# Two half-height products for the remainder rows of the last layer's first two matrices, on one Trainium2 core

## What is computed

```python
def _moe2_ref(x, w_a, w_b, w_out):        # x 3072 x 320, w_a and w_b 320 x 1536, w_out 1536 x 320
    a = x @ w_a
    b = x @ w_b
    return (a * b @ w_out).astype(np.float32)
```

## Time and profile before

| what | value |
| --- | --- |
| median of 3 runs | 934.4 us (932.12 to 934.41) |
| the profiled execution's own time | 929.12 us |
| its span, first to last instruction | 927.4 us |
| granted TensorE clock, mean of the span | 0.948 of full speed |
| TensorE busy | 811.5 us, 88% of the span |
| DVE busy | 612.4 us, 66% |
| ACT busy / POOL busy | 287.4 us / 168.8 us |
| matmuls of `wide` on wa and wb | 480 + 288 for each of the two |
| chain that ended last, by engine | PE 50%, DVE 18%, ACT 4%, DMA 4%, issue 3%, POOL 2% |

### The profile page before, as it was taken

One profiled execution on the slowest core, in us unless ns is written; L12 is line 12 of the kernel. 1 busy time (PEld: TensorE's weight loads), 2 busy tenths in 40 slices (PEclk: granted clock), 3 DMA queues, 4 the chain that ended last, 5 costly groups with the idle time before them and its releaser, 6 DMA issues.

```text
span 927.4 us, 16639 instructions
## 1 busy us (share of the span) xinstructions
PE 811.5 (88%) x5858; PEld 754.2 (81%) x5858; DVE 612.4 (66%) x1756; ACT 287.4 (31%) x538; POOL 168.8 (18%) x195
## 2 busy tenths in 40 slices
PE   1999999214699899989998999999899989999995
PEld 0999998213589888988898899889888989989995
DVE  7788898677657766785677657766766683364221
ACT  4444441302233422341234124312522342243221
POOL 6666565171000110010011001100110011011001
PEclk9999999555989999999999999999999999999998
DMA  4866661603202200220032004101300120050000
GB/s 113 251 212 207 212 200 37 204 0 115 74 22 84 85 22 1 63 84 21 0 100 68 0 0 132 35 1 44 102 21 0 63 83 22 1 146 23 1 1 21
DMA packets 51624, 66.63 MB, mean 72 GB/s; under 512 B 6376, under 2 KB 42232, under 8 KB 51576
## 3 DMA queue, kind: packets, MB, share of 16 engines
q1 hardware_dynamic: 37352, 50.31, 17.6%
q0 software_dynamic: 2368, 7.88, 3.0%
q10 hardware_dynamic: 11856, 7.87, 2.8%
HBM read 57.88 MB, written 8.16 MB: 71 GB/s over the span
## 4 chain that ended last, share of the span: by engine, by line
PE 50%; DVE 18%; ACT 4%; DMA 4%; issue 3%; POOL 2%; DVEq 0%; ACTq 0%; POOLq 0%
PE psA L897 20%; PE acc L920 11%; PE psB L897 9%; PE acc L947 7%; DMA xg<-xs_dram,idx_g 4%; DVE at_slot L1293 3%; DVE cmp L1155 2%; DVE ab L1375 2%; POOL xg L852 2%; ACT ab_hi L1120 2%; DVE ab_lo L1379 1%; PE psT L978 1%; PE psT L959 1%; ACT a_sb L1127 1%; PE psT L967 1%
## 5 line engine op out<-in xcount | busy, mean ns | idle before, releaser
L897 PE MATMUL psA<-x_hi,wa 128*128 128x384 f32 x480 | 138.5, 354 | 0.5 <-DVE x_lo L1400 0.4
L897 PE MATMUL psB<-x_hi,wb 128*128 128x384 f32 x480 | 132.0, 339 | 0.0
L852 POOL DMA_INDIRECT xg<-xs_dram,idx_g x24 | 25.1, 1045 | 462.2 <-DVE idx_g L1307 457.3
L1127 ACT COPY a_sb<-psA 128x384 f32<-128x384 f32 x96 | 46.0, 479 | 180.7 <-PE psB L897 180.7
L897 PE MATMUL psA<-x_lo,wa 128*128 128x384 f32 x288 | 98.0, 340 | 0.0
L897 PE MATMUL psB<-x_lo,wb 128*128 128x384 f32 x288 | 96.5, 335 | 0.0
L1375 DVE TENSOR_TENSOR ab<-a_sb,psB 128x384 f32<-128x384 f32 x96 | 53.0, 552 | 64.9 <-ACT a_sb L1127 64.0
L947 PE MATMUL acc<-wo_hi,ab_hi 128*128 128x320 f32 x288 | 93.1, 323 | 1.0 <-DVE ab_lo L1379 1.0
L947 PE MATMUL acc<-wo_hi,ab_lo 128*128 128x320 f32 x288 | 90.0, 313 | 0.0
L947 PE MATMUL acc<-wo_lo,ab_hi 128*128 128x320 f32 x288 | 90.0, 312 | 0.0
L897 PEld LDWEIGHTS psA<-x_hi,wa 128*128 128x128 f32 x480 | 85.3, 193 | 4.1 <-DVE x_lo L1400 2.1
(11 more groups left out here) (236 smaller groups left out, 1741.9 us busy)
## 6 DMA issues: line engine op xcount, KB each, us to landing
w_raw<-in_w_dram SPq DMA_DIRECT2D x32, 320.0 KB, 3.2
w_raw<-in_w_dram SPq DMA_DIRECT2D x32, 256.0 KB, 3.0
toks<-in_tok_dram SPq DMA_DIRECT2D x24, 324.0 KB, 3.5
qks<-in_qk_dram SPq DMA_DIRECT2D x48, 160.0 KB
w_raw<-in_w_dram SPq DMA_DIRECT2D x64, 64.0 KB, 2.8
gate<-in_tok_dram SPq DMA_DIRECT2D x6, 640.0 KB, 5.9
xs_dram<-y ACTq DMA_DIRECT2D x24, 160.0 KB, 3.3
qst<-in_qk_dram ACTq DMA_DIRECT2D x48, 60.0 KB
```

Of the source, the lines that this page charges most:

```text
L852: pool.indirect_dma_start(out=xg[:, t, 0:DM], out_offset=None, in_=xrows, in_offset=bass.IndirectOffsetOnAxis(ap=idx_g[:, t:t + 1], axis=0 ...
L897: last = pe.matmul(ps, w, x, start=(n == 0), stop=(n == len(steps) - 1))
L1127: act.copy(a_sb[g % 2][:, :], psA[g % 2][:, 0:CAP]).then_inc(sm["a_copied"], 1)
```

## The change

`wide` gets a flag by which it leaves out its last matmul (rest of the weights by x_lo); `pair` uses it for both matrices and then issues two matmuls of 64 rows: for wa on partitions 0 to 63, for wb on partitions 64 to 127. So that partitions 64 to 127 hold wb's high part, the low part of wb's rest is now written over partitions 0 to 63. `up`, which uses `wide` too, is unchanged. The product of the two low parts of the rest, which the matmul over 128 rows had computed as well, is left out for wa and wb now. The number of matmuls stays as it is.

```diff
+LOW_ROWS = (slice(HALF, P), slice(0, HALF))
 ...
         for i in range(2):
             pool.wait_ge(sm["wab_hi"], i + 1)
-            pool.tensor_tensor(second[i][64:P, 2, :], wab_raw[64:P, i, 2, :], f32(second[i][64:P, 2, :]), ALU.subtract).then_inc(sm["wab_lo"], 1)
+            rows_ = LOW_ROWS[i]
+            pool.tensor_tensor(second[i][rows_, 2, :], wab_raw[rows_, i, 2, :], f32(second[i][rows_, 2, :]), ALU.subtract).then_inc(sm["wab_lo"], 1)
 ...
-        def wide(ps, hi, lo, mixed, x_hi, x_lo, arrival=None, between=None):
+        def wide(ps, hi, lo, mixed, x_hi, x_lo, arrival=None, between=None, whole=True):
             steps = [(j, w(j), x[:, j, :]) for j in range(2) for w, x in ((hi, x_hi), (lo, x_hi), (hi, x_lo))]
-            steps += [(2, mixed, x_hi[:, 2, :]), (2, mixed, x_lo[:, 2, :])]
+            steps += [(2, mixed, x_hi[:, 2, :])]
+            if whole:
+                steps += [(2, mixed, x_lo[:, 2, :])]
 ...
-                last = pe.matmul(ps, w, x, start=(n == 0), stop=(n == len(steps) - 1))
+                last = pe.matmul(ps, w, x, start=(n == 0), stop=(whole and n == len(steps) - 1))
 ...
             for ps, w, between in ((psA, wa, between_a), (psB, wb, between_b)):
-                last = wide(ps[g % 2][:, 0:CAP], lambda j: w[:, j, c], lambda j: w[:, 3 + j, c], w[:, 2, c], x2_hi, x2_lo,
-                            3 * k if g == 0 and w is wa else None, between)
+                wide(ps[g % 2][:, 0:CAP], lambda j: w[:, j, c], lambda j: w[:, 3 + j, c], w[:, 2, c], x2_hi, x2_lo,
+                     3 * k if g == 0 and w is wa else None, between, False)
+            for ps, w, rows in ((psA, wa, slice(0, HALF)), (psB, wb, slice(HALF, P))):
+                last = pe.matmul(ps[g % 2][:, 0:CAP], w[rows, 2, c], x2_lo[rows, 2, :], start=False, stop=True)
             last.then_inc(sm["ab_mm"], 1)
```

## The result

The changed kernel takes 939.12 us (median of 6 runs, 936.42 to 941.99), the kernel before 934.45 (6 runs): a ratio of 1.0051, with a 95% interval of 1.003 to 1.0073. It is slower by 4.7 us, where 9.1 were forecast. The profiled execution took 936.42 us, with a span of 934.6.

The account below looks back on a forecast made before the run. The prediction took TensorE, busy for 88% of the span, as the bound. Pairs +11.3 us and clock -2.2 us gave +9.1 us, on a base of 934.4 us 943.5 us, range 936 to 954.

Parts of the forecast that it names:

- steps 1 to 3: End of each pair: both halves stream together, but each change of height empties the array; each pair 0.23 us longer.
- step 4: Expert turns: pairs 0 to 4 count in full, pair 5 with 0.03, later ones mostly shrink waits; 11.3 us in sum.
- step 5: Behind the wait after pair 10: shorter waits remove all four clock drops, -2.2 us, bounds 0 and -2.2.
- Halves together and no emptying: Last full matmul of each pair: halves overlap, array not emptied, each pair saves 0.166 us; 925.9 us, chance 0.09.
- One after the other: End of each pair: array emptied and halves run serially, each pair 0.39 us longer; 953.2 us, chance 0.12.
- Nothing taken up by the waits: All 96 pairs count with 0.23 us each, 22 us in all; 956.5 us, chance 0.06.
- No effect: End of each pair: halves pass through the array as full ones do, no overlap, no emptying; 934.4 us, chance 0.05.

Follow-up runs that it names:

- the kernel with pairs 6 to 10: Half-height products only in pairs 6 to 10 of turns with a successor, full ones elsewhere, against the kernel before: ratio 1.0011, in a second series 0.9992.
- the kernel with pairs 0 to 5: Half-height products only in pairs 0 to 5 of all eight turns, full ones in pairs 6 to 11, against the kernel before: 944.37 us, ratio 1.0095.
- the moved kernel: The two x_lo products stay at full height and only move to the end of the pair, against the kernel before: ratio 1.0014.
- experiment 2: The changed kernel with both half-height products on partitions 0 to 63, so they cannot share the array: 949.13 us, ratio 1.0196 to the kernel before.

## Why the prediction was right, and its size too large

**The pair (steps 1 to 3).** Right in the mechanism and in nearly each number: halves 0.01 us apart, 0.26 to 0.27 us to their load in all 96 pairs, 0.10 of uncovered load twice, 4.32 us a block; the project's record is 0.41 and not 0.44. The Trainium skill, TensorEngine Tiling (Array Packing), Key Properties, states that changing the tiling mode drains the engine. All 96 pairs agree with it. The Trainium skill, TensorE: Matmul & The Clock Gate, Part 3, has tiles on different rows run at the same time. The trace agrees (877.33 and 877.34); what it saves here, 0.17 us, is less than the 0.39 of a visit to half height.

**Where it reaches the end (step 4).** This is the step that was off in size: "pairs 0 to 4 count in full", 1.18 us in each turn with a search. The chain that ended last, in the changed kernel, where it leaves PE:

```profile
470.51 1.22 PE psB L901 x7
471.72 0.37 PE psA L942
472.10 0.02 PE psB L942
...
472.14 0.49 ACT a_sb L1133
```

Pair 0 of this turn began 2.87 us later than before (446.56 against 443.69), pair 5 ended 3.66 us later (472.12 against 468.46): the stretch grew by 0.79 and not 1.18. The difference is 3 x 0.13: pairs 1, 2 and 3 are followed by `gather_counts` and cost 0.10, which the prediction did not look at. The chain does leave PE at the end of pair 5, as forecast. Six turns of 0.8, turn 6 with 1.4 and the last turn with 2.5 (forecast 2.6) give 8.7 us in place of 11.3. The two profiles give 7.9: from pair 0 to the turned tile the seven turns together take 346.0 us in place of 340.6 (1.0 of the 5.4 in turn 6, where 1.4 were forecast), and the last turn, from pair 0 to the last project, 51.55 in place of 49.01. That PE's later arrival behind pair 5 costs nothing is shown by the kernel with pairs 6 to 10, which takes the time of the kernel before within its interval.

**The clock (step 5).** Right in kind, too small, and outside its own bound of -2.2. All drops went. From the end of the wait to the next turn's pair 0 the kernel before takes 0.55 to 0.73 us more than the changed one in the four turns with a drop, and the same within 0.04 in the other three: 2.7 us in all. In the kernel with pairs 0 to 5 all seven turns have the drop, and there the same stretch is 0.57 to 0.70 longer than in the changed kernel in six turns, and 1.55 in turn 6. And the profiled execution of before, with four drops, was a good one: its mean clock is 0.948, where the median of 20 other runs of this kernel is 0.944, and the moved kernel, whose time is the same, has five in its profile. The changed kernel has none at a mean clock of 0.954, so a drop is worth 0.0015 to 0.0016 of it, and 0.944 would be about six (an estimate from these numbers; the clock also differs ahead of the first pair). With 0.65 us each, five to six drops are 3.3 to 3.9 us. The 8.7 from above less that is 4.8 to 5.4; measured 4.7, interval 2.8 to 6.8.

**The profiled executions** differ by 7.3 us, more than the medians. Of that, 2.0 us lie ahead of the first pair (pair 0 of turn 0 starts at 269.95 us in place of 267.95), where the change does nothing but the POOL instruction at 185 us; in the other kernels this point lies between 268.4 and 274.3 us. From there to the last project it is 5.3 us, which is the 7.9 of the pairs less the 2.7 of the clock, to 0.1 us. So the forecast had the mechanism, and missed by two terms that erred to the same side: 11.3 for the pairs, where the profiles show 7.9, and 2.2 for the clock, where they show 2.7, and 3.3 to 3.9 is the estimate for a usual run. That its 9.1 is twice the measured 4.7 comes from both.

**The rivals.** Halves together and no emptying: excluded by the loads, and the moved kernel shows what its absence looks like. One after the other: that is experiment 2, whose second half starts 0.28 us behind the first record's start, 0.18 behind its columns; here it is 0.01. Nothing taken up by the waits: the wait shrank by 7.8 us. No effect: excluded by the interval.

## What to carry to other kernels

Matmuls of half height, two at a time, save a step of the array only for as long as it stays at that height: here one visit to half height costs 0.39 us with one half of 384 columns in it, and 0.22 with two, so three such couples in a row would be about where it begins to pay (an estimate, not run, from the 0.17 us that each couple saves and the 0.39 of the visit). If a visit can't be avoided, put it beside a small matmul whose successor has its weight load uncovered already, or in front of a wait. And a wait of the tensor engine can cost its clock behind it: here the half clock followed four of the seven waits of 2.1 to 3.0 us in the kernel before, and none of the seven of 1.1 to 1.7 us in the changed one. Cheap work in front of such a wait can be worth more than the work that one tries to save.

## What I had not expected

Ten useless matmuls a turn made the kernel 0.5% faster (ratio 0.995, 0.9931 to 0.997), and half as many half-height pairs lost about twice as much (9 us by the ratio against 4.7; 10.9 against 5.3 in the profiles, from the first pair on), because they lie on the chain, while those that would shorten the wait were missing. Filling the first search with 20 matmuls a round, 34.9 of 55 us busy, did not raise the clock from half.
